# Constant tiles multiplied in three waits of TensorE, in the first unit of a gated linear attention with two feed-forward blocks

## The chip, the cores and the metric

The kernel runs on one core of a Trainium2 chip. The metric is the device time of one execution in microseconds, as the median of several runs. The core's engines have a queue each and meet through semaphores: TensorE (PE, its weight loads PEld), VectorE (DVE), ScalarE (ACT), GpSimd (POOL) and SyncE (SP), which issues the DMAs.

## The reference

For 4 batches x 8 heads x 768 steps x 48 channels a complex diagonal recurrence is run: the gate `a_re + i a_im` is scaled so that its magnitude is at most 0.999, and then

```python
for t in range(S):
    new_re = ar * S_re - ai * S_im
    new_im = ar * S_im + ai * S_re
    S_re, S_im = (new_re + k[t] outer v[t], new_im)
    y[t] = q[t] @ S_re
```

The 3072 x 384 result goes through `elu(x @ w_in) @ w_out` (384 to 2048 to 384) and then `max(x @ w1, x @ w2, x @ w3) @ w_fin` (384 to 768 to 384). All of it is float32.

## The kernel before

The sequence is cut into six chunks of 128 steps. Within a chunk the recurrence is attention with a causal mask, with q and k scaled by the running decay and turned by the running angle; between chunks a state of 48 x 48 for each head is carried. A unit is two of the four batches of one chunk (12 units; n counts single rows of batch, two to a unit: "row a" and "row b"). ACT, POOL and DVE make the logarithms, the scans, the sines and the turned q and k (`rotate_q`, `rotate_k`, lines 945 to 961; `rotate_k` raises the semaphore `kpd`). SP stores q and k to memory and loads them back with channels in the partitions (`store_k`, `load_kt`, `load_qt`). On PE a row then takes `scores` (L1141), `k_rows` (L1130, transposes of k), `outputs` (L1167, y) and `increment` (L1151, the state's increment). Their results go through a ring of three PSUM banks (5 to 7), so that each of them can wait until an earlier tile has been copied out by ACT or DVE (`masked`, L963; `x_high`, L716; `x_low`, L997; `state_add`, L973; `k_rows` on ACT, L706).

The first feed-forward block runs in groups g: `first(g)` (L1190) into banks 0 and 1, an exponential on ACT (`exp_g`), two passes on DVE (`elu_g`), a high part on ACT (`high_g`) and a low part on POOL (`low_g`), then `second(g)` (L1209), which adds into banks 2 to 4. A float32 product is made of three matmuls on high and low parts in fp32r (`three`, L1125); the attention's matmuls are plain float32, and the trace shows two MATMUL instructions for each of them. The weights are split likewise by `w_in_high`, `w_out_high` (ACT), `w_in_low` (DVE, L1019) and `w_out_low` (POOL, L561).

The order of every engine's queue is written out: the tables `AT_FIRST`, `AT_SECOND` and `AT` give for each step of a unit its place x, and each engine's `attention(x)` issues what falls due at x. Before the first group all places up to 15 run; for unit 0 that is on PE: `scores(0)`, `k_rows(0)`, `outputs(0)`, `increment(0)`, `scores(1)`, `k_rows(1)`, `outputs(1)`, `increment(1)`, and then `first(0)`. The second block (`chunk`, L1264) follows when all groups are done.

Of the kernel before, what the change touches and what calls it, by code (L numbers as in the profile page):

```python
# [18 lines left out]
def build(nc, q, k, v, a_re, a_im, w_in, w_out, w1, w2, w3, w_fin, out):  # L19
    P = 128  # L20
    NC, _, B, W = q.shape
    _, C1, DM = w_out.shape
    F2 = w1.shape[2]
    D = 48
# [22 lines left out]
    T = B * P  # L47
# [56 lines left out]
    with ctx:  # L104
        def sb(name, shape, dt=f32, c=ctx):
            return c.enter_context(nc.sbuf_tensor(name, shape, dt))

        def sem(name):
            return ctx.enter_context(nc.semaphore(name))
# [6 lines left out]
        ident = sb("ident", [P, P])  # L116
        mask = sb("mask", [P, P])
        restart = sb("restart", [P, PAIR * W])
# [85 lines left out]
        bank = [ctx.enter_context(nc.psum_tensor(f"bank{n}", [P, 512], f32)) for n in range(8)]  # L204
# [27 lines left out]
        qpd, kpd = sem("q_rotated"), sem("k_rotated")  # L232
# [41 lines left out]
        def tile_of(g):  # L274

            if g < C1:
                t, j = divmod(g, CH)
                return t, j, slice(t * HALF, (t + 1) * HALF)
            t, j = divmod(g, C1)
            return t + 1, j, slice(0, T)  # L280

        def begins(t):
            return CH * t if t < 2 else C1 * (t - 1)

        def chunk_of_tile(t):
            return max(t - 1, 0)

        def keeps(n):
            return n < (NU - UPC) * PAIR
# [7 lines left out]
        for x in range(FIRST_POS, LAST_POS):  # L297
            for what in PIECES:
                u = at(x, what)
                if u is not None:  # L300
                    n = PAIR * u + (what[-1] == "b")
# [4 lines left out]
        def filling(pe, what, n):  # L306
            z = place[what, n]
            if z >= RING:
                pe.wait_ge(free[z % RING], z // RING)
            return bank[ATT + z % RING], full[z % RING]  # L310
# [6 lines left out]
        def emptied(eng, what, n):  # L317
            z = place[what, n]
            eng.wait_ge(free[z % RING], z // RING + 1)
# [801 lines left out]
        def _(pe):  # L1121
            def mm(dst, lhsT, rhs, start, stop):
                return nc.tensor.matmul(dst, lhsT, rhs, start=start, stop=stop)  # L1123

            def three(dst, wh, wl, ah, al, start, stop):  # L1125
                mm(dst, wh, ah, start, False)
                mm(dst, wh, al, False, False)
                return mm(dst, wl, ah, False, stop)

            def k_rows(n):  # L1130
                if not keeps(n):
                    return
                for z in range(2):
                    dst, done = filling(pe, f"kr{z}", n)
                    if z == 0:
                        pe.wait_ge(l_kt[n % 2], 16 * (n // 2 + 1))
                    for h in range(HB):
                        last = nc.tensor.transpose(dst[:, h * D2:(h + 1) * D2], kt[:, n % 2, HB * z + h, :], ident[0:D2, 0:D2])  # L1138
                    last.then_inc(done, 1)

            def scores(n):  # L1141
                pe.wait_ge(l_qt[n % 2], 16 * (n // 2 + 1))
                pe.wait_ge(l_kt[n % 2], 16 * (n // 2 + 1))
                for z in range(2):
                    dst, done = filling(pe, f"s{z}", n)
                    for h in range(HB):
                        last = mm(dst[:, h * P:(h + 1) * P], kt[:, n % 2, HB * z + h, :], qt[:, n % 2, HB * z + h, :],
                                  True, True)
                    last.then_inc(done, 1)
# [40 lines left out]
            def first(g):  # L1190
                t, j, tok = tile_of(g)
                i = chunk_of_tile(t)
                r = i % 2
                if g == begins(t):
                    emptied(pe, "y", B * i + B - 1 if t >= 2 else PAIR * t + 1)
                if g >= 2:
                    pe.wait_ge(elu, g - 1)
                if t == 0 and j % 2 == 0:
                    pe.wait_ge(wlo, j // 2 + 1)
                for z in range(2 if t < 2 else 1):  # L1200
                    c = 2 * j + z if t < 2 else j
                    dst = bank[g % 2][:, z * HALF:(z + 1) * HALF] if t < 2 else bank[g % 2][:, :]
                    cols = slice(c % 4 * P, (c % 4 + 1) * P)
                    for kk in range(KC):
                        last = three(dst, wih[:, c // 4, kk, cols], wil[:, c // 4, kk, cols],
                                     xh[:, r, kk, tok], xl[:, r, kk, tok], kk == 0, kk == KC - 1)
                last.then_inc(up, 1)
# [22 lines left out]
            def attention(x):  # L1230
                def now(what):
                    return at(x, what) is not None

                if now("kr_a"):
                    k_rows(PAIR * at(x, "kr_a"))
                if now("kr_b"):
                    k_rows(PAIR * at(x, "kr_b") + 1)
                if now("s_a"):
                    scores(PAIR * at(x, "s_a"))
                if now("s_b"):  # L1240
                    scores(PAIR * at(x, "s_b") + 1)
                if now("y_a"):
                    outputs(PAIR * at(x, "y_a"))
                if now("y_b"):
                    outputs(PAIR * at(x, "y_b") + 1)
                if now("inc_a"):
                    increment(PAIR * at(x, "inc_a"))
                if now("inc_b"):
                    increment(PAIR * at(x, "inc_b") + 1)
# [3 lines left out]
            for g in range(NG + AHEAD):  # L1253
                if g < NG:
                    first(g)
                    for x in after(2 * g):
                        attention(x)
                if g >= AHEAD:
                    second(g - AHEAD)
                if g < NG:  # L1260
                    for x in after(2 * g + 1):
                        attention(x)
# [24 lines left out]
            for i in range(NT):  # L1287
# [8 lines left out]
                for z in range(SUB):  # L1296
                    n = SUB * i + z
# [45 lines left out]
```

## Time and profile before

| | |
|---|---|
| median of 3 runs | 932.74 us (931.1 to 932.78) |
| the profiled execution | 932.65 us, span of its instructions 930.9 us |
| mean granted clock of TensorE | 0.981 |
| PE busy, weight loads busy | 847.4 us (91%), 734.5 us (79%) |
| DVE, ACT, POOL busy | 517.6, 419.5, 373.0 us |
| chain that ended last, by engine | PE 74%, issue 9%, DVE 7%, POOL 5%, ACT 3% |

Busy time is the time in which an engine has an instruction running. A chain is read backwards from the last instruction, each time to what released it. The granted clock is 1.00 at 2.4 GHz and 0.50 at 1.2 GHz; a mean between them says for what part of a stretch it was at either. PE's instructions overlap, so that a group of them is best read by where the next group starts.

### The profile page before, as it was taken

The numbers are of one execution on the slowest core, as the hardware profiler recorded it, in microseconds if no ns is written. First come the engines' busy times: TensorE is split into PE (matmuls) and PEld (weight loads), VectorE is DVE, ScalarE is ACT, GpSimd is POOL, SyncE is SP. The second block draws the span as 40 slices with busy tenths as digits, with TensorE's granted clock in tenths as the row PEclk, the third lists the DMA queues.
The fourth block names the chain that finished last, engine by engine and source line by source line (L and its number), as shares of the span: only waits on it lengthen the run. The fifth ranks groups of instructions, "written<-read, shape, count | busy, mean of one in ns | idle before, by whom it ended". The sixth has DMA issues, their size and how long they took to land.

```text
span 930.9 us, 14390 instructions
## 1 busy us (share of the span) xinstructions
PE 847.4 (91%) x5692; PEld 734.5 (79%) x5692; DVE 517.6 (56%) x702; ACT 419.5 (45%) x613; POOL 373.0 (40%) x272
## 2 busy tenths in 40 slices
PE   0067789899999999999999999999999999999997
PEld 0067789888888888888878888878888989898987
DVE  4858887788797878787878643553212121212020
ACT  6745746466666666666575423432121121112121
POOL 3544654444545454636454522465222131303120
PEclk9997898899999999999999999999999999999999
DMA  5396143435252625262524326003010102000000
GB/s 223 88 281 195 35 123 105 139 104 176 84 167 60 202 64 182 63 205 61 174 78 147 107 59 247 1 1 119 1 69 0 68 1 69 1 35 1 35 0 35
DMA packets 70723, 88.45 MB, mean 95 GB/s; under 512 B 15360, under 2 KB 55296, under 8 KB 70144
## 3 DMA queue, kind: packets, MB, share of 16 engines
q1 hardware_dynamic: 70656, 87.53, 30.1%
q8 instruction: 45, 0.74, 0.3%
q14 instruction: 22, 0.18, 0.1%
HBM read 59.13 MB, written 28.39 MB: 94 GB/s over the span
## 4 chain that ended last, share of the span: by engine, by line
PE 74%; issue 9%; DVE 7%; POOL 5%; ACT 3%; DMA 1%; POOLq 0%; SPq 0%; DVEq 0%; ACTq 0%
PE bank L1123 73%; POOL t L514 1%; DVE ge L862 1%; DVE t L868 1%; ACT t L633 1%; DVE t L862 1%; PE bank L1138 1%; POOL gl L517 1%; DVE qp L868 1%; POOL hl L517 1%; DVE ge L865 1%; POOL wol L517 1%; POOL qd L514 1%; POOL kd L514 1%; DVE kp L868 0%
## 5 line engine op out<-in xcount | busy, mean ns | idle before, releaser
L517 POOL TENSOR_TENSOR gl<-ge,gh 128x512 fp32r<-128x512 f32 x96 | 131.1, 1366 | 146.1 <-ACT gh L633 146.1
L868 DVE TENSOR_TENSOR hm<-bank,hm 128x512 f32<-128x512 f32 x72 | 49.8, 692 | 226.6 <-PE bank L1123 224.7
L1123 PE MATMUL bank<-xh,wih 128*128 128x512 f32 (+1 forms) x336 | 126.9, 378 | 9.7 <-DVE xl L868 9.7
L517 POOL TENSOR_TENSOR hl<-hm,hh 128x512 fp32r<-128x512 f32 x36 | 46.5, 1292 | 205.8 <-ACT hh L633 205.8
L1123 PE MATMUL bank<-gh,woh 128*128 128x512 f32 (+1 forms) x336 | 124.2, 370 | 5.2 <-POOL gl L517 4.8
L1123 PE MATMUL bank<-xh,wal 128*128 128x512 f32 x324 | 126.2, 389 | 0.0
L1123 PE MATMUL bank<-xl,wah 128*128 128x512 f32 x324 | 126.2, 389 | 0.0
L1123 PE MATMUL bank<-xh,wah 128*128 128x512 f32 x324 | 126.1, 389 | 0.0
L1123 PE MATMUL bank<-xh,wil 128*128 128x512 f32 (+1 forms) x336 | 122.2, 364 | 0.0
L1123 PE MATMUL bank<-xl,wih 128*128 128x512 f32 (+1 forms) x336 | 122.0, 363 | 0.0
L1123 PE MATMUL bank<-gl,woh 128*128 128x512 f32 (+1 forms) x336 | 121.6, 362 | 0.0
L1123 PE MATMUL bank<-gh,wol 128*128 128x512 f32 (+1 forms) x336 | 121.5, 362 | 0.0
L862 DVE TENSOR_SCALAR ge<-ge 128x512 f32<-128x512 f32 x96 | 70.9, 738 | 59.9 <-ACT ge L633 59.8
L1123 PE MATMUL bank<-qt,kt 96*128 96x128 f32 x384 | 53.0, 297 | 52.5 <-DMA kt<-k_cols 48.4
L633 ACT ACTIVATE gh<-ge 128x512 fp32r<-128x512 f32 x96 | 60.5, 630 | 87.9 <-DVE ge L865 87.6
L633 ACT ACTIVATE ge<-bank 128x512 f32<-128x512 f32 x96 | 57.1, 595 | 93.8 <-PE bank L1123 84.8
L1123 PEld LDWEIGHTS bank<-qt,kt 96*128 96x128 f32 x384 | 51.9, 212 | 54.0 <-issue 52.8
L514 POOL TENSOR_TENSOR qd<-qd,cs 128x384 f32<-128x384 f32 x24 | 41.6, 1732 | 119.9 <-ACT sn L633 119.9
L633 ACT ACTIVATE t<-t 128x768 f32<-128x768 f32 x96 | 80.7, 841 | 10.5 <-DVE t L865 4.8
L1123 PEld LDWEIGHTS bank<-xh,wih 128*128 128x128 f32 x336 | 64.9, 193 | 22.8 <-DVE xl L868 11.4
L633 ACT ACTIVATE hh<-hm 128x512 fp32r<-128x512 f32 x36 | 22.7, 631 | 129.2 <-DVE hm L868 129.2
L1123 PEld LDWEIGHTS bank<-gh,woh 128*128 128x128 f32 x336 | 64.2, 191 | 18.4 <-POOL gl L517 6.1
(83 smaller groups left out, 1681.8 us busy)
## 6 DMA issues: line engine op xcount, KB each, us to landing
q_cols<-qp SPq DMA_DIRECT2D x24, 384.0 KB, 2.8
k_cols<-kp SPq DMA_DIRECT2D x24, 384.0 KB, 3.0
qt<-q_cols SPq DMA_DIRECT2D x24, 384.0 KB, 3.7
kt<-k_cols SPq DMA_DIRECT2D x24, 384.0 KB, 3.9
vv<-in_v SPq DMA_DIRECT2D x12, 448.0 KB, 5.5
ar<-in_a_re SPq DMA_DIRECT2D x12, 384.0 KB, 3.6
ai<-in_a_im SPq DMA_DIRECT2D x12, 384.0 KB, 4.2
qd<-in_q SPq DMA_DIRECT2D x12, 384.0 KB, 4.2
```

What stands on the lines that cost most here:

```text
L514: return nc.gpsimd.tensor_tensor(dst, a, b, op)
L517: return nc.gpsimd.tensor_tensor(dst, whole, high.bitcast(f32), ALU.subtract)
L633: return nc.scalar.activation(dst, src, f, **kw)
L862: return nc.vector.tensor_scalar(dst, src, s1_, s2_, op0, op1)
L865: return nc.vector.scalar_tensor_tensor(out=dst, in0=a, scalar=s, in1=b, op0=op0, op1=op1)
L868: return nc.vector.tensor_tensor(dst, a, b, op)
L1123: return nc.tensor.matmul(dst, lhsT, rhs, start=start, stop=stop)
L1138: last = nc.tensor.transpose(dst[:, h * D2:(h + 1) * D2], kt[:, n % 2, HB * z + h, :], ident[0:D2, 0:D2])
```

## The change

A helper `hold(count)` is added to PE's program: `count` float32 matmuls of the 128x128 identity with a 128x512 part of the constant tile `restart` (ones, and a zero at each slice's start), all into bank 2, each one overwriting the last. Nobody reads that result: the first real use of bank 2 starts with an overwriting matmul too. It is called in three places, all in the first unit: 10 of them ahead of the scores of row a (after a new wait for `kpd`, the first turned k), 5 ahead of the k rows of row a, and 4 at the head of the first group's product.

```diff
+            def hold(count):
+
+                for _ in range(count):
+                    mm(bank[2][:, :], ident[:, :], restart[:, 0:T], True, True)
+
             def k_rows(n):
                 if not keeps(n):
                     return
+                if n == 0:
+                    hold(5)
                 for z in range(2):
                     dst, done = filling(pe, f"kr{z}", n)
...
             def scores(n):
+                if n == 0:
+                    pe.wait_ge(kpd, 1)
+                    hold(10)
                 pe.wait_ge(l_qt[n % 2], 16 * (n // 2 + 1))
                 pe.wait_ge(l_kt[n % 2], 16 * (n // 2 + 1))
...
                 r = i % 2
+                if g == 0:
+                    hold(4)
                 if g == begins(t):
                     emptied(pe, "y", B * i + B - 1 if t >= 2 else PAIR * t + 1)
```

## Rows read from the trace of the kernel before

**Rows 1.** Busy time by stretch: length, then PE, PEld, DVE, ACT, POOL, clock, DMA, GB/s

```profile
200.00:300.00 100.00, 98.01 (x766) 83.59 (x767) 78.07 (x112) 64.25 (x93) 48.55 (x37) 1.00 0.39 117
```

**Rows 2.** Waits of PE over the span: total, times, longest

```profile
PE bank L1123 <- DMA kt<-k_cols: 48.4, 1, 48.4
PE bank L1123 <- DVE xl L868: 9.7, 5, 6.1
PE bank L1138 <- DVE sc L868: 8.8, 3, 5.6
```

**Rows 3.** Timeline of PE: start, length, instructions, and idle time before them

```profile
48.42 3.76 PE L1123 MATMUL bank<-qt,kt 96*128 96x128 f32 x16 [48.42 <-DMA kt<-k_cols]
...
58.41 0.90 PE L1138 MATMUL bank<-ident,kt 96*128 96x96 f32 x4 [5.59 <-DVE sc L868]
59.24 1.94 PE L1123 MATMUL bank<-sc,vv 128*32 128x128 f32 x32
61.10 2.80 PE L1123 MATMUL bank<-vv,kr 128*96 128x64 f32 x16
63.70 3.75 PE L1123 MATMUL bank<-qt,kt 96*128 96x128 f32 x16
...
70.64 1.56 PE L1123 MATMUL bank<-vv,kr 128*96 128x64 f32 x16
78.31 0.58 PE L1123 MATMUL bank<-xh,wih 128*128 128x256 f32 x1 [6.12 <-DVE xl L868]
...
82.32 2.75 PE L1123 MATMUL bank<-qt,kt 96*128 96x128 f32 x16
...
87.83 1.08 PE L1123 MATMUL bank<-sc,vv 128*32 128x128 f32 x32
...
92.45 1.95 PE L1123 MATMUL bank<-qt,kt 96*128 96x128 f32 x16
...
109.90 0.58 PE L1123 MATMUL bank<-gh,woh 128*128 128x256 f32 x1 [4.14 <-POOL gl L517]
```

**Rows 4.** Stretches of 2 us, columns as in rows 1

```profile
72.00:74.00 2.00, 0.19 (x3) 0.07 (x1) 1.99 (x3) 0.03 (x1) 0.00 (x0) 0.94 0.75 237
...
82.00:84.00 2.00, 2.00 (x11) 2.00 (x11) 1.97 (x3) 1.44 (x2) 0.00 (x0) 0.50 0.93 285
...
106.00:108.00 2.00, 0.00 (x0) 0.00 (x0) 1.97 (x2) 0.00 (x0) 2.00 (x3) 0.97 0.64 246
...
114.00:116.00 2.00, 2.00 (x20) 2.00 (x19) 1.00 (x2) 1.94 (x3) 2.00 (x1) 0.82 0.00 0
```

**Rows 5.** The idle time of PE at 200 us, and PE's busy time and clock there

```profile
201.38 0.50 PE L1123 MATMUL bank<-xh,wih 128*128 128x512 f32 x1 [1.85 <-DVE xl L868]
...
200.00:202.00 2.00, 0.62 (x3) 1.00 0.02 0
```

**Rows 6.** Timeline of DVE

```profile
36.85 0.55 DVE L868 TENSOR_TENSOR kp<-kd,sn 128x384 f32<-128x384 f32 x1
...
57.67 1.28 DVE L868 TENSOR_TENSOR sc<-bank,mask 128x512 f32<-128x512 f32 x2
...
64.80 2.23 DVE L868 TENSOR_TENSOR kp<-kd,cs 128x384 f32<-128x384 f32 x1 [0.24 <-DVE st L980]
...
77.71 0.55 DVE L868 TENSOR_TENSOR xl<-bank,xh 128x384 fp32r<-128x384 f32 x1
...
83.20 0.42 DVE L862 TENSOR_SCALAR ge<-ge 128x512 f32<-128x512 f32 x1
```

**Rows 7.** Timelines of ACT and POOL, after y of row a and after the first product

```profile
61.63 1.48 ACT L633 ACTIVATE woh<-wor 128x1536 fp32r<-128x1536 f32 x1
...
82.56 0.60 ACT L633 ACTIVATE ge<-bank 128x512 f32<-128x512 f32 x1 [1.93 <-PE bank L1123]
...
63.18 3.43 POOL L517 TENSOR_TENSOR wol<-wor,woh 128x1536 fp32r<-128x1536 f32 x1 [9.32 <-ACT woh L633]
...
84.60 3.50 POOL L517 TENSOR_TENSOR wol<-wor,woh 128x1536 fp32r<-128x1536 f32 x1 [8.57 <-ACT woh L633]
```

## The prediction, made before the changed kernel was run

> **What bounds the kernel now.** I read the stretches first. From 200 us on PE is the bound: 98.01 of 100 us busy between 200 and 300 at the full clock [rows 1]. The change touches only what comes before, where PE waits. The list of PE's waits shows three in the first unit [rows 2]: 48.4 us for the k columns of row a, 5.6 us for DVE's masked scores, 6.1 us for DVE's x low part. The changed kernel multiplies in just these. It does no work in them that anyone needs, so only one thing can come of it: that TensorE's clock is higher in what follows.
>
> The timeline of PE is next [rows 3]. The same 16 score instructions take 3.76 and 3.75 us at 48.42 and 63.70, and 1.95 us at 92.45; y takes 1.94 at 59.24 and 1.08 at 87.83. So up to about 70 us PE runs at the 1.2 GHz level by its durations (the clock column reads 1.00 there, before the first change that it records at 73.8; I go by durations). At 78.31 the first product again runs low, and the clock is back at 84.0, since the stretch 82 to 84 shows 0.50 to its end [rows 4].
>
> **What the clock does, by rows.** It falls after short idle times: PE is idle from 72.2 (70.64 + 1.56) and the clock falls at 73.76 (0.94 over 72 to 74: 0.24 us at half), after 1.6 us; idle from 105.76, falls at 107.88, after 2.1 us [rows 3, 4]. An idle time of 1.85 us at 200 did not bring it down [rows 5]. It rises 5.7 us after dense matmuls began (78.31 to 84.0) and 4.8 us after (109.90 to 114.72) [rows 3, 4]. With attention work alone it took longer: 58.41 to about 70.
>
> **The price of a hold.** No row has a float32 matmul with 512 columns. The score instructions have 128 columns and take 3.75/16 = 0.234 us low and 1.95/16 = 0.122 us high; a hold is two instructions with four times the columns, so at most 8 x 0.234 = 1.88 and 8 x 0.122 = 0.98 us. I take 1.72 and 0.90, somewhat less, since a part of the short instruction is fixed.
>
> **Part 1, ten ahead of the scores of row a.** The wait for `kpd` ends with DVE's second k product, 36.85 + 0.55 = 37.40 [rows 6]. PE had nothing to do before 48.42 anyway, and behind this wait stands only the work that waits for the k columns. With the rise after 5.3 us: 3.1 holds low (5.3 us), 6.9 high (6.2 us), end at 48.9, 0.5 us behind the columns. Bounds: no rise in the ten, 17.2 us, end 54.6; rise after 12 us, end 52.1. The scores then take 1.95 instead of 3.76: done at 50.9 instead of 52.2. That gain goes to nobody. DVE masks them at 57.67, right behind the q products that precede it in its queue, and needed them by then in either kernel.
>
> **Part 2, five ahead of the k rows.** 5 x 0.90 = 4.5 us, 50.9 to 55.4; half of the k rows follows (0.45), and then PE waits for DVE's first masked half as before, until 58.41: an idle time of 2.55 us in place of 5.59. By the two falls above that is long enough (1.6 and 2.1 us). If the clock stayed high, the second half of the k rows would save 0.45, y 1.94 - 1.08 = 0.86 and the increment 2.80 - 1.56 = 1.24 us: 2.55 in all [rows 3]. If it falls before 58.41, nothing; if it falls within y, about half of the first two, 0.6.
>
> What of that reaches the end goes through one place. ACT copies y, then splits a part of w_out (61.63), and POOL's low part starts behind it at 63.18 for 3.43 us [rows 7]. DVE's next k product (64.80) needs 2.23 us where it needs 0.55 alone: it sits out the POOL instruction [rows 6]. So the k product of unit 1 ends about 0.4 us behind POOL, and moves with the end of y (at most 1.3 us), not with the increment. Behind it: the store of k, the next k product, w_in's low part, and x low at 77.71, which releases the first product at 78.31.
>
> The Trainium skill has this as a rule (SBUF — State Buffer, "Who interferes with whom"): the pair of ports that DVE and GpSimd share is an exclusive lock, and the second to start blocks until the first is done. The 2.23 us at 64.80 agree with it.
>
> **Part 3, four ahead of the first product.** They start at 72.2 or a little before. High all through: 3.6 us, end 75.8, and 2.5 us idle to 78.31; low all through: 6.9 us, end 79.1, 0.8 us late. The clock stands high from about 70.4 before, so I take the first, with a fair chance that it falls in the 2.5 us. If it stays high, the 18 matmuls of the first product (78.31 to 82.32, 4.0 us) take half, and the scores behind it 1.95 instead of 2.75: PE is 2.8 us ahead at 84.8. Who gains? DVE: its first elu pass starts at 83.20 with no idle time before it, behind w_in's low part, and so cannot start sooner [rows 6]. So of this part I pass on nothing.
>
> **The sum.** Profiled execution 932.65 us. Part 1: 0. Part 2: between 0 and 1.3 us at the end of y, taken as 0.7 of it: the clock falls late rather than early. Part 3: 0 to -0.8. The DVE and ACT queues between 84 and 200 pass on a shift with gains and losses of their own. Sum -0.7: 931.95, against a median 0.09 above the profiled execution; I say 932.0 us. Its own range is 930.9 to 933.4.
>
> **Rivals.**
>
> A, the clock stays high from 49 to 84 us. For it: 1.85 us idle left it up [rows 5], and both idle times left are shorter than the ones before (5.59, 6.12). Against: falls after 1.6 and 2.1 us. Then y is 1.3 us sooner; the k product, its store and loads start 1.1 us sooner, at a time when the transfers of weights tail off, so that the store lands up to 1 us faster too, and the next k and q products get ahead of POOL's square. x low comes some 2.5 us sooner. Time 930.1 (range 929.2 to 930.9). The Trainium skill's table (TensorE: Matmul & The Clock Gate, "Why this matters for your kernels") warns only of idle gaps between bursts longer than either of those left here; by it this rival would be the forecast. The fall at 73.76, 1.6 us into an idle time, speaks against it.
>
> B, slower, by the fast first product. If the first product ends near 80.4, ACT's exponential (82.56) runs 1.9 us sooner, and the w_out split behind it too. POOL's low part, 84.60 for 3.50 us [rows 7], then starts at 82.7, before DVE's elu pass at 83.20 [rows 6] instead of after it. That pass reads SBUF alone and would sit out POOL until about 86.2; the high part, the next exponential and the next elu slip 2 to 2.8 us. In return a later DVE pass is free of POOL. Place: 83.2 us; decides when the first product is over 1.4 us sooner against DVE. Net price 0 to +2.8, taken as +2.2: 934.9. For it: such a block of an elu pass is what 64.80 shows for k. Against: it needs part 3 to work without part 2 moving DVE.
>
> C, slower, the holds do not raise the clock. The scores at 63.70 ran low for all of 3.75 us though dense. Then ten holds end at 54.6, scores 58.4, five holds 67.0, k rows, y and increment at 73.5, 9.6 us behind 63.9: 942.2.
>
> D, nothing: the clock falls in both gaps. 932.7.
>
> **Chances.** Forecast (a part of the saving) 0.40, A 0.27, B 0.10, C 0.03, D 0.20. This kernel's measurement tells about 0.2%, 1.9 us, from no change. Faster by more than that: most of A and a little of the forecast, 0.30. Slower: most of B, C, and a tail of D, 0.12. Same 0.58. The range takes A's and B's ends: 929.4 to 934.8.
>
> **What would show each step.** Ten holds as 20 instructions from 37.4 to about 49, spaced 0.86 and later 0.45 us. Scores in about 2 us. If the k rows at 58.4 take 0.9 us for four, the clock fell (D); y in 1.1 and increment in 1.6 us mean A. The start of the first product: 78.3 for D, 77.6 forecast, near 76 for A. For B: an elu pass near 83 of over 2 us. I am wrong if k's store of unit 1 does not move with y, or if the changed kernel's PE idle time between 100 and 200 moves by itself by over 2 us.

## The result, and the profile after

The changed kernel took 933.85 us against 931.65 us before (medians of ten executions each): ratio 1.0021, 95% interval 1.0011 to 1.0031. It is slower by 2.2 us, where the forecast was 0.7 us less than before. The time lies inside the range of 929.4 to 934.8 us, near the 934.9 us of rival B, which was given 0.10.

The execution that was profiled first is not typical: 931.41 us (span 929.6) where the nine others took 933.0 to 935.1. It shows the case of the forecast (931.95 us). PE's longest waits in it answer to [rows 2] (total, times, longest):

```profile
PE bank L1123 <- DVE kp L868: 37.5, 1, 37.5
PE bank L1145 <- DVE sc L868: 6.5, 4, 2.7
PE bank L1123 <- DVE xl L868: 5.9, 5, 2.2
```

The timeline of PE in that execution, beside [rows 3]; `restart,ident` are the holds:

```profile
37.53 11.78 PE L1123 MATMUL bank<-restart,ident 128*128 128x512 f32 x20 [37.53 <-DVE kp L868]
49.15 1.95 PE L1123 MATMUL bank<-qt,kt 96*128 96x128 f32 x16
50.94 4.46 PE L1123 MATMUL bank<-restart,ident 128*128 128x512 f32 x10
...
58.40 0.55 PE L1145 MATMUL bank<-ident,kt 96*128 96x96 f32 x4 [2.67 <-DVE sc L868]
59.20 1.08 PE L1123 MATMUL bank<-sc,vv 128*32 128x128 f32 x32 [0.25 <-DVE sc L868]
60.28 2.52 PE L1123 MATMUL bank<-vv,kr 128*96 128x64 f32 x16
62.60 3.75 PE L1123 MATMUL bank<-qt,kt 96*128 96x128 f32 x16
...
71.73 3.67 PE L1123 MATMUL bank<-restart,ident 128*128 128x512 f32 x8
77.64 0.58 PE L1123 MATMUL bank<-xh,wih 128*128 128x256 f32 x1 [2.25 <-DVE xl L868]
81.39 1.95 PE L1123 MATMUL bank<-qt,kt 96*128 96x128 f32 x16
...
108.86 0.58 PE L1123 MATMUL bank<-gh,woh 128*128 128x256 f32 x1 [4.13 <-POOL gl L517]
```

The scores of row a and y run high (1.95 and 1.08 us), the scores of row b low (3.75). The clock between them, and around the first product, in stretches of 2 us (length, PE busy, clock, DMA, GB/s), beside [rows 4]:

```profile
60.00:62.00 2.00, 2.00 (x25) 0.64 1.03 285
...
76.00:78.00 2.00, 0.35 (x1) 0.91 0.98 258
...
80.00:82.00 2.00, 2.00 (x15) 0.74 0.82 195
```

0.64 over 60 to 62 is a fall at 60.6 (1.44 us at half), 0.91 over 76 to 78 one at 77.6, just as the first product begins, and 0.74 a rise at 81.0. So each of the two idle times that were left (2.67 and 2.25 us) was followed by a fall, and the first product ran mostly low. DVE in this execution, beside [rows 6]: the k product of unit 1, x low, and the first elu pass.

```profile
63.70 2.44 DVE L868 TENSOR_TENSOR kp<-kd,cs 128x384 f32<-128x384 f32 x1 [0.24 <-DVE st L980]
...
77.04 0.55 DVE L868 TENSOR_TENSOR xl<-bank,xh 128x384 fp32r<-128x384 f32 x1
...
82.54 0.42 DVE L862 TENSOR_SCALAR ge<-ge 128x512 f32<-128x512 f32 x1
```

All of them are 0.7 to 1.1 us sooner than in [rows 6], and the wait for POOL at 108.86 ends 1.0 us sooner than in [rows 3].

### The profile page after: what moved, and what is told of

Read it like the earlier page. It is cut to its first block, busy times and chain, and to the rows that moved or that the text cites. A ratio compares the mean times of both kernels' runs of the same rounds, so it can differ in the third digit from the quotient of the medians.

```text
span 929.6 us, 14467 instructions
## 1 busy us (share of the span) xinstructions
PE 861.9 (93%) x5730; PEld 738.0 (79%) x5730; DVE 516.3 (56%) x702; ACT 419.8 (45%) x613; POOL 373.4 (40%) x272
## 4 chain that ended last, share of the span: by engine, by line
PE 73%; issue 9%; DVE 7%; POOL 5%; ACT 3%; DMA 1%; POOLq 0%; SPq 0%; DVEq 0%; ACTq 0%
PE bank L1123 72%; DVE ge L862 1%; POOL t L514 1%; DVE t L868 1%; ACT t L633 1%; DVE t L862 1%; DVE ge L865 1%; POOL gl L517 1%; PE bank L1145 1%; DVE qp L868 1%; POOL wol L517 1%; POOL hl L517 1%; POOL qd L514 1%; POOL kd L514 1%; DMA k_cols<-kp 0%
## 5 line engine op out<-in xcount | busy, mean ns | idle before, releaser
L1123 PEld LDWEIGHTS bank<-xh,wil 128*128 128x128 f32 x336 | 64.3, 191 | 9.9
L1123 PEld LDWEIGHTS bank<-gh,wol 128*128 128x128 f32 x336 | 64.0, 190 | 9.7
```

## The experiments

Medians of 6 to 12 executions, with the kernel before on the same chip. The ratio is the recorded one with its interval; it is not the quotient of the two medians and differs from it by up to 0.0010. The last two columns are of each one's profiled execution: the length of DVE's first elu pass, and the moment at which PE's wait for POOL's `gl` near 110 us ends.

| kernel | us | before | ratio, interval | elu pass | PE at |
|---|---|---|---|---|---|
| before, profiled | | | | 0.42 | 109.90 |
| changed, again | 934.32 | 931.15 | 1.0033, 1.0016 to 1.0051 | 3.69 | 112.65 |
| holds 10 and 5 only | 930.32 | 931.15 | 0.9997, 0.9988 to 1.0006 | 0.42 | 109.55 |
| 4 ahead of the first product only | 934.38 | 931.15 | 1.0030, 1.0016 to 1.0044 | 0.42 | 109.01 |
| 10, 5 and 7 | 934.24 | 931.15 | 1.0023, 1.0007 to 1.0039 | 3.68 | 114.03 |
| no holds, w_out split sooner | 934.41 | 931.26 | 1.0044, 1.0029 to 1.0059 | 3.69 | 113.52 |
| no holds, w_out split later | 933.18 | 931.26 | 1.0024, 1.0013 to 1.0035 | 0.42 | 111.12 |
| 10, 5, 4, split later | 934.29 | 931.26 | 1.0041, 1.0027 to 1.0055 | 0.42 | 112.56 |
| 10, 5, 7, split later | 934.23 | 931.26 | 1.0039, 1.0024 to 1.0055 | 0.42 | 112.66 |
| 10, 5, 4, POOL waits for the elu pass | 930.99 | 930.95 | 0.9999, 0.9988 to 1.0010 | 0.42 | 108.56 |
| 10, 5, 7, POOL waits | 931.06 | 930.95 | 1.0004, 0.9995 to 1.0012 | 0.43 | 110.14 |
| 10, 8, 7, POOL waits | 932.79 | 930.95 | 1.0012, 0.9998 to 1.0026 | 0.42 | 109.08 |
| no holds, POOL waits | 931.63 | 930.95 | 1.0009, 0.9999 to 1.0019 | 0.42 | 109.54 |
| no holds but 3 in the last wait | 929.91 | 931.00 | 0.9987, 0.9976 to 0.9999 | 0.42 | 109.29 |
| 10, 5, 4, POOL waits, 3 in the last wait | 929.80 | 931.00 | 0.9985, 0.9974 to 0.9996 | 0.42 | 108.89 |

**Which of the three places costs.** First the changed kernel once more, unchanged:

> The changed kernel once more, for a second profile, since the profiled execution of the first (931.4 us) lies under nine of its ten times (933.0 to 935.1). Theory P (product: when the clock stays high into the first product, ACT splits w_out sooner and POOL's low part starts ahead of DVE's first elu pass, which then sits it out): about 934 us, and a profile of such an execution shows the first product in about 2.2 us, an elu pass of over 2 us near 82 us. Theory E (early: the holds ahead of the scores and k rows cost): about 934 us, with the first product late or the k product of unit 1 late in the profile.

Then each part alone. Holds ahead of the scores and k rows of row a only:

```diff
                 if g == 0:
-                    hold(4)
```

> Only the holds ahead of the scores and the k rows of row a (10 and 5); the four ahead of the first product are left out. Theory P: nothing is lost, a part of y's gain arrives: 0 to 1 us faster than before (ratio 0.999 to 1.000). Theory E: the whole loss is here, ratio 1.002.

Only those ahead of the first product:

```diff
                 if n == 0:
-                    hold(5)
...
                 if n == 0:
-                    pe.wait_ge(kpd, 1)
-                    hold(10)
```

> Only the four holds ahead of the first product. Theory P: the whole loss, ratio about 1.002 (2 us). Theory E: ratio 1.000.

And more of them there:

```diff
                 if g == 0:
-                    hold(4)
+                    hold(7)
```

> The changed kernel with seven holds instead of four ahead of the first product, so that no idle time is left before it and the clock is high in it in every execution; seven end near 78 us, within half a microsecond of x low. Theory P: at least the loss of the changed kernel, in every execution, 934 us or more, with the long elu pass near 83 us in any profile. A third theory (L: the loss comes from executions in which the clock fell before the first product): the loss goes, 931 us or less.

The whole loss is with the holds ahead of the first product (1.0030 alone, 0.9997 without). E falls. L, that the executions with a low first product were the dear ones, is not borne out: seven holds lose about as much in the median (1.0023). But P's "in every execution" was wrong too, since three of those twelve took 931.2 us or less. The profiled execution with four holds alone (932.84 us) shows no collision: its first product ran low for the most part and the elu pass took 0.42 us. The second profile of the changed kernel has the other case. PE in it:

```profile
59.07 1.93 PE L1123 MATMUL bank<-sc,vv 128*32 128x128 f32 x32
...
73.23 4.68 PE L1123 MATMUL bank<-restart,ident 128*128 128x512 f32 x8
77.91 0.39 PE L1123 MATMUL bank<-xh,wih 128*128 128x256 f32 x1
...
80.39 2.02 PE L1123 MATMUL bank<-qt,kt 96*128 96x128 f32 x16
...
112.65 0.45 PE L1123 MATMUL bank<-gh,woh 128*128 128x256 f32 x1 [3.53 <-POOL gl L517]
```

The holds run up to the product here, since the increment ahead of them had run low and the holds could not start before 73.2; the first product takes 2.5 us up to the scores, instead of 4.0. Note the first row: y ran low, so that part 2 of the prediction gave nothing here. And the other engines in that execution, behind 80 us:

```profile
80.36 0.60 ACT L633 ACTIVATE ge<-bank 128x512 f32<-128x512 f32 x1
80.86 1.48 ACT L633 ACTIVATE woh<-wor 128x1536 fp32r<-128x1536 f32 x1
...
82.41 3.80 POOL L517 TENSOR_TENSOR wol<-wor,woh 128x1536 fp32r<-128x1536 f32 x1 [6.77 <-ACT woh L633]
...
82.81 3.69 DVE L862 TENSOR_SCALAR ge<-ge 128x512 f32<-128x512 f32 x1
...
87.26 0.63 ACT L633 ACTIVATE gh<-ge 128x512 fp32r<-128x512 f32 x1 [4.93 <-DVE ge L865]
```

What matters is the order of the starts. ACT's exponential comes 2.2 us sooner than in [rows 7], its w_out part follows at once, and POOL starts at 82.41, 0.4 us ahead of DVE's pass, instead of at 84.60. DVE's pass of 0.42 us then ends 0.3 us behind POOL's 3.8. ACT's high part waits 4.9 us for DVE, the low part and the second product follow it, and PE's wait near 110 us ends at 112.65 instead of 109.90. The Trainium skill (SBUF — State Buffer, "Who interferes with whom") says that the one which starts first keeps the shared ports for its whole instruction and the other blocks; this row agrees, with 3.69 us for 0.42.

**The order alone, with no hold.** This takes the clock out of the question:

```diff
-        "w_out_high": (-14, 8, 16, 25)
+        "w_out_high": (-14, 8, 15, 25)
```

> The kernel before, without any hold, with ACT's third part of w_out one place sooner, ahead of the first exponential instead of behind it. ACT is free from about 80.6 us, so POOL's low part starts near 82.2 instead of 84.6, with the clock and the first product as they were. Theory P says that it is this order alone that costs: DVE's first elu pass takes over 3 us, and the kernel is 2 to 4 us slower than before (934 us). Theory C (the cost of the changed kernel comes from the clock or from a faster PE by itself, and the long elu pass only stands beside it): no change, 931 us.

It costs 3.1 us by the medians. The engines between 80 and 84 us, and PE near 110:

```profile
80.26 1.47 ACT L633 ACTIVATE woh<-wor 128x1536 fp32r<-128x1536 f32 x1
...
81.81 4.53 POOL L517 TENSOR_TENSOR wol<-wor,woh 128x1536 fp32r<-128x1536 f32 x1 [6.05 <-ACT woh L633]
...
82.94 3.69 DVE L862 TENSOR_SCALAR ge<-ge 128x512 f32<-128x512 f32 x1
...
113.52 0.39 PE L1123 MATMUL bank<-gh,woh 128*128 128x256 f32 x1 [3.54 <-POOL gl L517]
```

The first product there starts at 78.03 and its exponential at 82.28; in the control below, which also has no holds, they start at 78.03 and 82.27. So the collision is sufficient for the loss: theory P holds, C falls. POOL's part is longer too (4.53 us for 3.5). It started while DVE's low part of w_in was running (81.27, 1.75 us), which reads two tiles in SBUF; that fits the same block the other way round, but no run tests it.

**A mend that failed.** The part was put behind the first group's high part, with 4 and with 7 holds and, as a control, with none:

```diff
-        "w_out_high": (-14, 8, 16, 25)
+        "w_out_high": (-14, 8, 17, 25)
```

> The changed kernel (10, 5 and 4 holds) with ACT's third part of w_out behind the first group's high part, so that POOL's low part starts behind DVE's first elu pass whatever the first product takes. Theory P: the loss goes, 929 to 931 us in every execution, the elu pass near 83 us takes 0.42 us. Theory C: 934 us as before.

> Seven holds ahead of the first product (clock high in it in every execution) with the same later place of the w_out part. Theory P: the loss goes and some of the faster first product arrives, 928 to 930.5 us. Theory C: 934 us or more.

> Control: the kernel before, without holds, with the later place of the w_out part. It tells what the later place does by itself. Theory P: the collision wasn't there, so within 1 us of before, 930 to 932 us; if it is itself 2 us faster, the gain of the two runs with holds is not the holds'.

All three expectations of P were wrong, the control's too (1.0024). The first elu pass is free, but the collision has only moved. In the control, DVE's second elu pass and POOL:

```profile
88.24 3.31 DVE L862 TENSOR_SCALAR ge<-ge 128x512 f32<-128x512 f32 x1 [2.16 <-ACT ge L633]
```

```profile
87.80 3.47 POOL L517 TENSOR_TENSOR wol<-wor,woh 128x1536 fp32r<-128x1536 f32 x1 [12.05 <-ACT woh L633]
```

POOL starts at 87.80, 0.44 us ahead of it. ACT's exponential is late besides, since the split now stands before it. That is the same mechanism once more, and no test of the holds. With the holds this order costs about 1 us more than without them (934.29 and 934.23 against 933.18); in both of those profiles PE also waits 2.4 to 2.5 us for ACT's copy of the k rows near 89 us, against 0.35 in the control.

**A mend of the order alone.** Every place as it was, one wait more on POOL:

```diff
             def w_out_low(z):
                 pool.wait_ge(wohi, z + 1)
+                if z == 2:
+                    pool.wait_ge(em1, 1)
```

> The changed kernel, every order as it was, and one wait more: POOL's low part of the third w_out piece waits until the first pass of DVE's first elu is done. Theory P: the loss of the changed kernel goes, since POOL starts at about 83.7 us instead of 82.4, behind that pass, and sooner than the 84.6 of before: 930 to 931 us, ratio 0.998 to 1.000, the first elu pass 0.42 us. Theory C (the faster first product costs in another way): 934 us.

> Seven holds ahead of the first product and the same wait. Clock high in the first product in every execution. Theory P: as fast as any, 929.5 to 930.5 us, ratio about 0.999, and less scatter than the changed kernel. Theory C: 934 us.

> Control: the kernel before with the same wait alone. POOL's part starts at 84.6 there, after the elu pass's end at 83.6, so the wait is over before it is reached: no change, 931 us, ratio 0.9995 to 1.0005, by every theory.

> 10, 8 and 7 holds and the wait: no idle time of over a microsecond is left to TensorE from 37.5 to 78 us, so that y and the k rows of row a run high too. y ends 1 to 1.3 us sooner than at the low clock, the k product of unit 1 with it. If that reaches the end: 0.5 to 1.5 us under the run with 10, 5, 7 and the wait, 929 us. If it is taken up by the store of k and the loads behind it: no difference between the two.

With the wait the changed kernel loses nothing: 0.9999, against 1.0033 and 1.0021 without. Its lines are two further down; the first product there ran high (77.90, scores at 80.15), and between 80 and 84 us DVE and POOL stand in the old order:

```profile
82.81 0.42 DVE L864 TENSOR_SCALAR ge<-ge 128x512 f32<-128x512 f32 x1
...
83.37 3.47 POOL L517 TENSOR_TENSOR wol<-wor,woh 128x1536 fp32r<-128x1536 f32 x1 [7.74 <-DVE ge L864]
```

So where the order is kept there is no loss. But no version gained, though theory P had expected it of the longer holds. The control (1.0009) lies above the 0.9995 to 1.0005 that was expected, and within its noise of no change. The version with 10, 8 and 7 holds was expected at 929 us and took 932.79, its interval just reaching no change; why it is not as fast as the one with 10, 5 and 7 (931.06) stays open. In its profile y in fact ran high (59.04, 1.08 us) and DVE's k product of unit 1 ended 1.1 us sooner than before, yet x low was only 0.6 us sooner. The seven holds missed their aim in two profiled executions: with the increment ahead of them low, they held the product back until 80.1 and 79.1 us, though x low was ready at 78.2 and 77.7. That they make the clock high in every execution at no delay, as I had written, was wrong.

**Where a lead goes at the end.** The profiled execution of the changed kernel led by 2.8 us at PE's last wait and by 1.3 at the end. PE's last wait and the clock behind it in the kernel before:

```profile
913.90 0.69 PE L1123 MATMUL bank<-wfh,hh 128*128 128x384 f32 x1 [2.85 <-POOL hl L517]
```

```profile
910.00:916.00 6.00, 3.15 (x12) 0.79 0.01 3
916.00:920.00 4.00, 4.00 (x22) 0.89 0.00 0
```

and in the changed kernel:

```profile
911.10 0.69 PE L1123 MATMUL bank<-wfh,hh 128*128 128x384 f32 x1 [2.85 <-POOL hl L517]
```

```profile
910.00:916.00 6.00, 4.90 (x15) 0.54 0.00 0
916.00:920.00 4.00, 4.00 (x21) 0.84 0.13 49
```

The clock was low for longer there: 6.8 us of the ten between 910 and 920, against 3.4. From the end of the last wait to the end of the span it took 18.5 us, against 17.0. Two kernels keep the clock up over that wait, with three holds in a bank that is free by then:

```diff
+                if i == NT - 1:
+                    pe.wait_ge(mx2, C2 * NT - 1)
+                    for _ in range(3):
+                        mm(bank[5][:, :], ident[:, :], restart[:, 0:T], True, True)
                 pe.wait_ge(hlo, C2 * (i + 1))
```

> The kernel before with three holds in PE's last wait (2.85 us, for POOL's last low part) and none in the first unit. Theory T (tail: the clock falls in or after that wait and the last 72 matmuls run low in part): the last product is done 1.4 to 3 us sooner, 928.5 to 930 us, ratio 0.997 to 0.9985, and no part of the last product shows the lower clock. Rival (the tail is long for another reason, or the holds end late): no change or up to 1 us slower.

> Holds 10, 5 and 4 in the first unit, POOL's third w_out part behind DVE's first elu pass, and three holds in PE's last wait. Theory T: 927.5 to 929.5 us, at most 1 us under the kernel with the three last holds alone if the first-unit holds are worth anything with the order mended. Rival: equal to the run with the last holds alone, so that the first-unit holds bring nothing.

Both are faster than the kernel before, by 1.1 and 1.2 us (intervals below 1 both). In the first of them:

```profile
910.70 2.74 PE L1123 MATMUL bank<-restart,ident 128*128 128x512 f32 x6
913.72 0.44 PE L1123 MATMUL bank<-wfh,hh 128*128 128x384 f32 x1 [0.28 <-POOL hl L517]
```

```profile
910.00:916.00 6.00, 5.71 (x23) 1.00 0.01 3
916.00:920.00 4.00, 4.00 (x25) 1.00 0.14 49
```

Nothing of the last product up to 920 us is low. From the end of the last wait to the end of the span it takes 15.7 us, and 15.6 in the other kernel, against 17.0 before: 1.3 us, which fits the 1.1 and 1.2 us of the medians. That is less than the 1.4 to 3 us that were expected. Between the two kernels no difference can be told (929.91 and 929.80): the 19 holds in the first unit bring nothing that can be told even with the order mended. These two are the versions that beat both kernels; the simpler one has the three last holds alone.

**Where the scatter comes from.** Single executions with the last holds still differ by 2.7 us and more (928.5 to 931.2, 928.2 to 931.6). The sixteen profiles show three places, the same in kernels with and without holds. PE starts scores near 178 us after an idle time of 2.3 to 3.9 us, and multiplies again near 200 us after one of 1.3 to 2.6. Two kernels without holds differ there; first the kernel before, whose row near 200 us is in [rows 5], then the one in which POOL waits:

```profile
178.09 3.75 PE L1123 MATMUL bank<-qt,kt 96*128 96x128 f32 x16 [3.86 <-issue]
```

```profile
176.78 2.02 PE L1125 MATMUL bank<-qt,kt 96*128 96x128 f32 x16 [3.03 <-issue]
...
199.19 0.71 PE L1125 MATMUL bank<-xh,wih 128*128 128x512 f32 x1 [2.60 <-DVE xl L870]
```

In the four profiles with a mean clock of 0.83 over 170 to 190 us (the kernel before among them), the way from PE's wait near 110 to the one near 200 took 91.2 to 92.3 us; in the twelve others (0.91 to 1.00) 89.0 to 90.4. In the five with an idle time of 2.15 to 2.60 near 200 the clock fell behind it (0.88 over 196 to 210), and from there to the last wait it took 714.0 to 714.2 us; in the eleven with 1.29 to 1.87 it stayed high, and it took 712.4 to 712.6. The last product is the third place: 18.5 us in two profiles, 16.9 to 17.3 in the twelve others without holds there. So a lead or a lag of 2 us at 110 can be undone in a single profile. The profiled execution with four holds alone led by 0.9 us there, had 0.83 near 180, and reached the last wait at the same 913.90 as the kernel before.

## Why the prediction was wrong, point by point

- **The price of a hold and part 1 were right.** Ten holds took 11.8 us to the scores at 49.15 in the first profile (11.5 and 48.9 forecast) and 10.2 to 10.8 us in the others, five took 4.46 us (4.5). The scores ran high, and what they gained reached nobody, since DVE's mask came at its old time.
- **Part 2 came in one profile of nine.** In the first, the idle time was 2.67 us (2.55 forecast), y ran high, the clock fell during the increment, and the k product of unit 1 and x low came 0.9 and 0.7 us sooner (0.7 forecast). In the eight other profiles with 10 and 5 holds the ten were done sooner, the idle time before the second half of the k rows was 3.2 to 3.4 us, and y ran low (1.93 or 1.94 us, as before). So the 0.7 us that the sum was made of was there only now and then; in the timed runs the two early parts together are worth 0.9997, no difference that can be told.
- **Part 3 is the step that failed:** "So of this part I pass on nothing". Its premise was right: the elu pass cannot start sooner, and it hardly did (82.81 in the dear execution, 83.20 before). But it can end later. I had worked that out as rival B, at the right place, 83.2 us, by the right engines, and gave it 0.10, with the condition that part 3 works "without part 2 moving DVE". That condition was met: in the two profiles with the collision and holds y ran low, part 2 gave nothing, and DVE's pass stood at 82.81 and 82.98, about where it stands in kernels without holds (82.91 to 83.20), while the exponential came 2.0 to 2.2 us sooner. Where part 2 did work, in the first profile, the first product ran low. With four holds the clock was high in the first product in four profiles of six. That nine of the ten first executions were slow fits a collision that is the common case, though only profiled executions show it.
- **B's size:** +2.2 us forecast. The measured time lies inside the range only because B's end had been taken into it; the forecast's own range (930.9 to 933.4) misses it. The order alone costs 3.1 us, the changed kernel 2.2 and 3.2 in its two sets. The second part of B, that a later DVE pass is free of POOL in return, is right too (at 88.66 that pass takes 1.01 us instead of 2.7), and does not make up for it.
- **Rival A** did not come. Where the clock was kept high on purpose (10, 8, 7 holds), 1.1 us at the k product became 0.6 at x low, and nothing at the end. By the table of the Trainium skill (TensorE: Matmul & The Clock Gate, "Why this matters for your kernels"), which warns only of longer idle times, it would have been the forecast. The measurements decide against it: idle times of 2.67 and 2.25 us were each followed by a fall, and so were those of 2.15 to 2.60 near 200 us, though one of 3.03 us near 178 us was not (the scores behind it took 2.02 us).
- **What stays open:** how often the clock is high in the first product of a timed execution, and whether holds in the first unit change how often it falls near 178 and 200 us, since only profiled executions show either.

## What to carry to other kernels

A wait that is filled to keep TensorE fast is worth what follows it on the path, and nothing more: price it by who waits for the faster work, and ask what that engine will then start sooner. Where two engines block each other, the order in which they start is part of the schedule, and a faster third engine can turn it round; hold such an order by a wait. The place to fill is a wait with nothing but TensorE's work behind it: here the last one, where three matmuls gave what nineteen in the first unit did not. And before one profile is read as the effect of a change, look at where the clock fell in it, and compare it with a second profile of the same kernel.

## What the runs showed of the hardware

A float32 matmul of 128x512 is two instructions of about 0.45 us each at the high clock (five holds, ten instructions, 4.46 us). A DVE pass of 0.42 us took 3.69 us behind a POOL instruction that had started 0.4 us sooner, and a POOL instruction of 3.5 us took 4.53 when it started 0.5 us behind a DVE instruction of 1.75 us with two inputs in SBUF; DVE passes that read PSUM (sc, 0.69 us, beside the POOL instruction at 84.60 in the kernel before) took no longer. The kernel before differs between its executions by 3.7 to 4.4 us in 931 (three sets of 23 to 35), the changed one by 7.6 (12 executions). The profiles show where: from PE's wait near 110 us to the one near 200 the longest takes 3.4 us more than the shortest, behind the idle time near 200 us 1.6, in the last product 1.5, each with a lower granted clock in the longer ones. So one profiled execution, here 2.4 us under its kernel's median, can show a case that is not the common one.
